# A fused mixing and two-layer kernel: TensorE's program without a loop, and the softmax of the mixing weights in pieces over two blocks

## What is computed

```python
# 1. mixing: softmax over K=7 taps for each token and each of 8 heads, then a causal weighted sum
w = exp(weight_gen - max_k(weight_gen)); w = w / (sum_k(w) + 1e-9)     # [B, S, 8, 7]
x[t, head, :] = sum_k w[t, head, k] * x_pad[t + k, head, :]            # 24 features a head
# 2. layer 1, d_ff = 2048: h = x @ w_in
P = a0 + a1*h + a2*h**2 + a3*h**3;  Q = 1 + |b0|*|h| + |b1|*h**2
x = (P / (Q + 1e-6)) @ w_out
# 3. layer 2, d_ff = 2048: h = x @ w_in2
y = (h * clip(h + 3, 0, 6) / 6) @ w_out2
```

## Time and profile before

| | us |
|---|---|
| median of 3 runs | 1297.59 |
| lowest and highest run | 1291.99, 1297.89 |
| profiled execution, its own time | 1295.64 |
| span of the profiled execution | 1293.9 |
| TensorE busy (matmuls) | 1198.3 |
| VectorE busy | 1204.2 |
| ScalarE busy | 1187.1 |
| GpSimd busy | 1091.9 |
| mean granted TensorE clock | 0.983 |

### The profile page before, as it was taken

The page is one execution under the profiler, slowest core; times in us unless marked ns, Lnnn a source line. Parts: engine busy times, 40 slices in busy tenths (PEclk is TensorE's granted clock), DMA queues, the critical chain, the costliest instruction groups (busy, mean ns, idle before and its releaser), DMA issues.

```text
span 1293.9 us, 19407 instructions
## 1 busy us (share of the span) xinstructions
PE 1198.3 (93%) x5128; PEld 967.6 (75%) x5128; DVE 1204.2 (93%) x1898; ACT 1187.1 (92%) x2221; POOL 1091.9 (84%) x817
## 2 busy tenths in 40 slices
PE   2456899999999999999899999999999999999998
PEld 1344678887888778887688878887788888888876
DVE  5689999999999999999899999999999999999932
ACT  3878999999999999999799999999999999999954
POOL 5878979897998979898797979989798989965554
PEclk9679999999999999999999999999999999999999
DMA  5443222321322322140223213123221302000000
GB/s 168 99 118 78 69 61 50 81 54 38 75 48 61 74 61 49 50 83 28 61 50 85 49 40 75 46 61 74 61 50 52 76 26 54 13 17 1 13 13 13
DMA packets 61464, 73.62 MB, mean 57 GB/s; under 512 B 15912, under 2 KB 42280, under 8 KB 61096
## 3 DMA queue, kind: packets, MB, share of 16 engines
q1 hardware_dynamic: 61352, 72.35, 24.2%
HBM read 56.44 MB, written 8.01 MB: 50 GB/s over the span
## 4 chain that ended last, share of the span: by engine, by line
PE 60%; DVE 22%; issue 11%; ACT 6%; DMA 1%; SPq 0%; POOLq 0%; POOL 0%; ACTq 0%; DVEq 0%
PE h L653 6%; PE h L657 6%; PE h L656 6%; PE h L654 6%; PE h L655 6%; PE acc L661 6%; PE acc L662 6%; PE acc L665 6%; PE acc L664 6%; PE acc L663 6%; DVE early L1031 5%; DVE early L1025 4%; DVE early L1056 4%; DVE early L1019 3%; DVE q_recip L1040 3%
## 5 line engine op out<-in xcount | busy, mean ns | idle before, releaser
L592 POOL TENSOR_TENSOR g_lo<-early,g_hi 128x512 fp32r<-128x512 f32 x256 | 333.3, 1302 | 116.2 <-ACT g_hi L847 107.2
L601 POOL TENSOR_TENSOR g_lo<-late,g_hi 128x512 fp32r<-128x512 f32 x256 | 333.4, 1303 | 23.7 <-ACT g_hi L867 23.7
L653 PE MATMUL h<-x_hi,w_in_hi 128*128 128x512 f32 x512 | 209.1, 408 | 64.1 <-DVE early L1056 61.7
L1064 DVE SCALAR_TENSOR_TENSOR late<-late,h 128x512 f32<-128x512 f32 x256 | 174.5, 682 | 42.8 <-ACT late L858 40.0
L661 PE MATMUL acc<-g_hi,w_out 128*128 128x512 f32 x512 | 202.6, 396 | 5.1 <-DVE late L1076 3.0
L654 PE MATMUL h<-x_lo,w_in_hi 128*128 128x512 f32 x512 | 202.1, 395 | 0.0
L657 PE MATMUL h<-x_tail_lo,w_in_tail 128*128 128x512 f32 x512 | 202.0, 394 | 0.0
L656 PE MATMUL h<-x_tail_hi,w_in_tail 128*128 128x512 f32 x512 | 201.7, 394 | 0.0
L655 PE MATMUL h<-x_hi,w_in_lo 128*128 128x512 f32 x512 | 201.7, 394 | 0.0
L662 PE MATMUL acc<-g_hi,w_out 128*128 128x512 f32 x512 | 201.2, 393 | 0.0
L663 PE MATMUL acc<-g_lo,w_out 128*128 128x512 f32 x512 | 200.7, 392 | 0.0
(11 more groups left out here) (87 smaller groups left out, 2464.2 us busy)
## 6 DMA issues: line engine op xcount, KB each, us to landing
mix_w<-mix_weights SPq DMA_DIRECT2D x75, 192.0 KB
mix_w<-mix_weights SPq DMA_DIRECT2D x75, 144.0 KB
x_win<-in_x SPq DMA_DIRECT2D x15, 393.0 KB, 3.4
mix_w<-mix_weights SPq DMA_DIRECT2D x60, 96.0 KB
mix_w<-mix_weights SPq DMA_DIRECT2D x60, 72.0 KB
out_y<-late SPq DMA_DIRECT2D x16, 256.0 KB, 2.0
x_tail_hi<-tail_hi SPq DMA_DIRECT2D x60, 64.0 KB, 2.0
x_tail_lo<-tail_lo SPq DMA_DIRECT2D x60, 64.0 KB, 2.0
```

Source lines behind the costliest of these rows:

```text
L592: nc.gpsimd.tensor_tensor(g1_lo[p][:, :], neg_g[p], g1_hi[p][:, :].bitcast(F32), ALU.subtract).then_inc(g1_lo_ready, 1)
L601: nc.gpsimd.tensor_tensor(g2_lo[p][:, :], gate[p], g2_hi[p][:, :].bitcast(F32), ALU.subtract).then_inc(g2_lo_ready, 1)
L653: pe.matmul(out[:, :], w_hi[:, cols], hi[:, :], start=True, stop=False)
```

## The change

TensorE's program is written out for all 18 segments, as the others are: `segments`, `Fori` and the register in the counts go.

The softmax of a part p from 3 on is spread over two segments. In the odd one before: maximum of a fourth of the part (16 tokens, 128x112 to 128x16) on VectorE at each of c=4, 6, 8 and 10, subtraction at c=13. In the even one: exp at c=0; the sum over taps on GpSimd, six additions of 128x64 at c=4 to 9 and the 1e-9 at c=10, each waiting for the one before it; the reciprocal on VectorE in two halves of 128x32 at c=12 and 13; the scaling at c=15. Part 2 is done in segment 0, with the scaling at c=1 of segment 1. SyncE loads a part behind the store of the one before it, no longer at the start of its own segment.

```diff
-        def segments(eng, segment):
-            for s in range(FIRST, LOOP_FROM):
-                segment(0, s)
-            with eng.Fori(0, LOOPS) as turn:
-                for s in range(LOOP_FROM, LOOP_FROM + LOOP_BLOCKS):
-                    segment(turn, s)
-            for s in range(LOOP_FROM + LOOP_BLOCKS * LOOPS, LAST + 1):
-                segment(0, s)
...
-            segments(pe, segment)
+            all_segments(segment)
...
-        def part_steps(s, at):
-            part = (s + 4) // 2
-            return {at: part} if s >= 0 and s % 2 == 0 and part < PARTS else {}
-
-        MAX_AT, SUB_AT, EXP_AT, SUM_AT, SCALE_AT = 7, 10, 10, 11, 14
+        EARLY_STEPS = {"max": {4: (0,), 6: (1,), 8: (2,), 10: (3,)}, "sub": {13: (0,)}}
+        LATE_STEPS = {"exp": {0: (0,)}, "sum": {4: (1,), 5: (2,), 6: (3,), 7: (4,), 8: (5,), 9: (6,), 10: (7,)},
+                      "recip": {12: (0,), 13: (1,)}, "scale": {15: (0,)}}
+        THIRD_EARLY = {"max": {6: (0, 1), 7: (2, 3)}, "sub": {10: (0,)}, "exp": {10: (0,)},
+                       "sum": {12: (1, 2, 3), 13: (4, 5, 6, 7)}, "recip": {14: (0,), 15: (1,)}}
+        THIRD_LATE = {"scale": {1: (0,)}}
+
+        def part_steps(s, step, c):
+            found = []
+            if s == 0:
+                found = [(2, THIRD_EARLY)]
+            elif s == 1:
+                found = [(2, THIRD_LATE), (3, EARLY_STEPS)]
+            elif s > 1:
+                found = [(s // 2 + 3, EARLY_STEPS) if s % 2 else (s // 2 + 2, LATE_STEPS)]
+            return [(part, k) for part, steps in found if part < PARTS for k in steps.get(step, {}).get(c, ())]
...
-                for part in part_steps(s, 0).values():
-                    if part == 2:
-
-                        sp.wait_ge(out_lo[1], 8)
-                    load_gen(part)
+                if s == 0:
+
+                    sp.wait_ge(out_lo[1], 8)
+                    load_gen(2)
...
-                for part in part_steps(s, 0).values():
+                part = s // 2 + 2
+                if s >= 0 and s % 2 == 0 and part < PARTS:
                     sp.wait_ge(gen_scaled, part + 1)
                     store_gen(part)
                     sp.wait_ge(gen_stored[part], 16 * H)
+                    if part + 1 < PARTS:
+                        load_gen(part + 1)
...
+            def sum_tap(part, k):
+                if k == 1:
+                    pool.wait_ge(gen_exp, part + 1)
+                else:
+                    pool.wait_ge(gen_sum, sum_count(part, k - 1))
+                stat = gen_stat(part)
+                if k == K:
+                    nc.gpsimd.tensor_scalar(stat, stat, 1e-9, None, ALU.add).then_inc(gen_sum, 1)
+                else:
+                    so_far = gen_w(part)[:, 0, :] if k == 1 else stat
+                    nc.gpsimd.tensor_tensor(stat, so_far, gen_w(part)[:, k, :], ALU.add).then_inc(gen_sum, 1)
...
+            def max_fourth(part, i):
+                if i == 0:
+                    dve.wait_ge(gen_loaded[part], 16)
+                cols = fourth(part_tokens(part), i)
+                dve.tensor_reduce(gen_stat(part)[:, cols], over_k(gen_w(part))[:, cols, :], AX_X,
+                                  ALU.max).then_inc(gen_max, 1)
+
+            def recip_half(part, half):
+                if half == 0:
+                    dve.wait_ge(gen_sum, sum_count(part))
+                n = part_tokens(part) // 2
+                stat = gen_stat(part)[:, half * n:(half + 1) * n]
+                dve.reciprocal(stat, stat).then_inc(gen_recip, 1)
```

More of the change, by code:

```diff
@@ L249, in build_program, with count @@
         x2_tail_lo_ready = sem("x2_tail_lo_ready")
-        def count(turn, per, block, more):
-            return turn * (LOOP_BLOCKS * per) + (block * per + more)
+        def count(per, block, more):
+            return block * per + more
         def all_segments(segment):
             for s in range(FIRST, LAST + 1):
-                segment(0, s)
-        def segments(eng, segment):
-            for s in range(FIRST, LOOP_FROM):
-                segment(0, s)
-            with eng.Fori(0, LOOPS) as turn:
-                for s in range(LOOP_FROM, LOOP_FROM + LOOP_BLOCKS):
-                    segment(turn, s)
-            for s in range(LOOP_FROM + LOOP_BLOCKS * LOOPS, LAST + 1):
-                segment(0, s)
+                segment(s)
         def has1(s, c, back=0):
@@ L409, in _ @@
             sp.wait_ge(gen_stored[0], 16 * H)
-            load_mix_w(0, 1, slice(0, A_TAPS), mix_w_a)
+            load_mix_w(1, slice(0, A_TAPS), mix_w_a)
             sp.wait_ge(in1_tail_lo, 4)
@@ L417, in _, with mix_done, copy_tail @@
             sp.wait_ge(gen_stored[1], 16 * H)
[L418 to L424, removed]
+            load_mix_w(1, slice(A_TAPS, K), mix_w_b)
+            def mix_done(blk, taps):
+                sp.wait_ge(mix_product_ready, count(K, blk - 1, taps))
+            def copy_tail(blk):
                 hi, lo = x1[blk % 2][2], x1[blk % 2][3]
-                sp.wait_ge(x1_tail_hi_ready, count(turn, 1, blk, 0))
+                sp.wait_ge(x1_tail_hi_ready, count(1, blk, 0))
                 for rows in (0, D2):
@@ L435, in copy_tail, with segment @@
                                      tail_lo[half * D2:(half + 1) * D2, :].bitcast(F32)).then_inc(tail_lo_copied, 16)
-            def segment(turn, s):
+            def segment(s):
                 if s == -1:
@@ L630, in prepare @@
                         split_out(1, i, (slot1, slot0)[i // 2])
[L631 to L632 removed]
+                    for part, _ in part_steps(s, "sub", c):
+                        subtract_max(part)
+                    for part, k in part_steps(s, "sum", c):
+                        sum_tap(part, k)
                     if n == 2:
                         scale(1)
[L635 to L636 removed]
+                    for part, _ in part_steps(s, "scale", c):
+                        scale(part)
                 for c in range(NC):
@@ L916, in prepare @@
                         exp_gen(1)
-                    if c in part_steps(s, EXP_AT):
-                        exp_gen(part_steps(s, EXP_AT)[c])
+                    for part, _ in part_steps(s, "exp", c):
+                        exp_gen(part)
                 for c in range(NC):
```

229 lines of the change are left out of this document (115 added, 114 removed).

## The result

The changed kernel takes 1279.26 us (median of 4 runs, 1277.9 to 1279.63) against 1294.79 (4 runs, 1291.76 to 1297.89). The ratio is 0.9885, with a 95% interval of 0.9867 to 0.9903. The forecast was 1277.5, with a range of 1271 to 1287. The profiled execution takes 1279.6 us against 1295.64, so 16.0 less where 18.4 were summed up. In a later comparison on another chip the same kernel gives 1277.97 us and a ratio of 0.9871 (0.9849 to 0.9893).

A forecast was written before the change was run, and what follows sets the result against it. TensorE, VectorE and GpSimd were taken as near full, handing work over each step. Five pairs 11.0, segment 0 1.7 and loop 5.7 make 18.4 us; 1295.64 - 18.4 = 1277.2, stated as 1277.5, range 1271 to 1287.

The forecast's parts named there:

- The loop, 5.7 us: TensorE's one backward jump, between segments 6 and 7: removing it gives back 5.7 us.
- The 0 taken as left: Straight-line code where the jump was: 0 of the 5.7 us remains, bounds 0 and 5.7.
- The pieces on VectorE, 1.5 us: Softmax work on VectorE per part: 3.27 us removed, four maxima and two half reciprocals added at 1.5 us.
- The pair, 146.7 us: Two segments, maximum to maximum: 148.9 us falls to 146.7, a gain of 2.2 us, bounds 2.5 and 0.9.
- the prediction's own three steps: Rule that each VectorE piece comes off its lead over TensorE three steps after the piece's own step.
- the walk: VectorE's lead over TensorE followed step by step: 146.4 us a pair with the new pieces, 148.6 with the old placement.
- The sum on GpSimd, 0: Seven added 128x64 operations at 0.3 us, 2.1 us per even segment: GpSimd's lead absorbs them, nobody waits.
- Waits and queues, 0: Waits of exp, additions and scaling, and SyncE's stores and loads: cost 0.
- Segment 0, 1.7 us: Part 2's softmax in segment 0: 1.8 us of TensorE waiting saved, 0.1 added for maxima, gain 1.7.
- rival of small operations with a high price of their own: Each small VectorE or GpSimd operation costs near 0.45 (or 0.59) us, a pair gives 0.9: 1284 us, chance 0.15.
- the rival of a gap that stays: Gap between segments 6 and 7 is no jump and stays, 5.7 us not won: 1283 us, chance 0.06.
- straight code holding up TensorE: Rival: long straight code outruns what fills TensorE's queue, 5.7 us per gap, slower than before: chance 0.03.

The follow-up runs named there:

- e1_straight: Kernel before with only TensorE's loop written out as straight code: 1290.65 us, ratio 0.997.
- e4_max_whole: Changed kernel with the maximum in one piece at c=7 of the odd segment, not four fourths: 1279.61 us, ratio 0.987.
- e7_max_late: Changed kernel with the maximum in one piece at c=12, subtraction at c=15, exp at c=1 of the even segment: 1276.51 us, ratio 0.9847.
- e6_sum_on_vector: Changed kernel with sum over taps, 1e-9 and reciprocal back on VectorE, together at c=11 of the even segment: 1288.5 us, ratio 0.995.
- e11_subtract_later: e10_halves_late with subtraction moved to c=1 of the even segment, exp to c=2, sum to c=5 to 11: 1278.33 us, ratio 0.9858.
- e10_halves_late: e7_max_late with its maximum cut in two halves, at c=12 and c=14 of the odd segment: 1300.66 us, ratio 1.0045.
- e5_add_on_vector: Changed kernel with the addition of 1e-9 on VectorE at c=12, ahead of the reciprocals, not on GpSimd: 1278.83 us.

## Why the prediction was right, step by step

The direction, the mechanism and the size came out. Of 18.4 us the profiled execution shows 16.0; the medians show 15.5, and 17.7 in the later comparison.

- **The loop, 5.7 us.** Right for the profiled execution (5.7 in e1_straight's comparison), and the place and the cause are shown by moving the jump. But it was one draw: over many runs the loop costs 4.1 us. The forecast used a single gap as if it were fixed, while the spread of the three runs shown, 6 us, already had room for the doubt. That did the forecast no harm, since it took the price of the dear jump off an execution that held this jump. The 0 taken as left was right.
- **The pieces on VectorE, 1.5 us.** Four fourths at 0.27 and two halves at 0.27 make 1.6. The line through two sizes of the reduction was good to 0.02 us an operation. The smaller estimate that the prediction drew from the Trainium skill (VectorE: DVE Perf Modes, The TRN2 errata), 0.18 us for a fourth and 0.9 for all six pieces, does not hold here: a fourth lasts 0.35 us, or 0.27 from start to start, and the six take 1.6.
- **The pair, 146.7 us.** Measured 146.8 to 146.9, with the predicted wait at its predicted step: 0.57 to 0.71 us at c=10 of odd segments against about 0.5, and none at c=13 of even ones, or at c=14, which by the prediction's own three steps is the place that the sum at c=11 had hit. The level itself, though, rests in part on a correction: the walk gave 146.4, and 0.3 was added because it lay 0.3 under the trace in both old cases. Five pairs gave 10.3 us, not 11.0. e4_max_whole, e7_max_late and e6_sum_on_vector came out within 0.2 us of the same walk, e11_subtract_later 0.6 beside it and e10_halves_late 5, both for waits that the walk didn't have; e7_max_late had its wait at c=4, where the walk had put it at c=5.
- **The sum on GpSimd, 0.** Right. 0.28 us an addition, and the least lead that I found was about 0.9 us in both kinds of segment, where 0.9 had been named for the odd and 1.3 for the even one. The even one was mis-sized, because at c=9 five additions lie ahead, and I had counted at c=7.
- **Waits and queues, 0.** Right: no computing engine waits for a load or a store more than before (SyncE's queue does stand for its own stores, 3.0 us at most), and GpSimd's new wait for the second half reciprocal, 0.8 us at most, lies in its slack.
- **Segment 0, 1.7 us.** The mis-sized term in the profiled execution: 0.8. The granted clock is lower in the start-up there, 0.72 and 0.83 in the two stretches of 10 us from 130 on where the kernel before had 0.85 and 1.00; the mean clock between 100 and 180 us is 0.91 and not 0.96. In the repeat of the same kernel it is 0.98, and segment 0 takes 72.07 us, 1.6 less than before. The start is a draw as well, and the first 109 us, for which nothing was summed, took 0.7 us more.

So the forecast missed by 2.4 us in the profiled execution: about 1.6 from the start, where the clock varies from run to run, and 0.7 in the pairs. The rival of small operations with a high price of their own falls by e5_add_on_vector and the rows above, the rival of a gap that stays falls by e1_straight, and no run showed straight code holding up TensorE.

## What to carry to other kernels

Where three engines are nearly full, follow the lead of one over the next from step to step. A piece of extra work costs what the lead lacks when it comes due, so its place counts more than its cutting: an uncut maximum at c=12 beat four fourths at c=4 to 10. Then look at every wait that the late engine feeds, not at the one that shows up today, at the other engines that feed the same wait, and at what is queued behind each new wait: a subtraction placed one step after its input in program order stood 5.7 us, since GpSimd was that far ahead of VectorE in its program. A loop's jump on a full TensorE is worth removing, but price it from many runs.

## What the runs showed of the hardware

- Over one backward jump on TensorE two matmuls started 1.5 to 4.2 us apart, in four profiled executions. At 3.5 and 4.2 us the granted clock fell to 0.60 over the next four us, which cost 1.8 us more; at 1.5 and 2.6 us it stayed at 1.0. All told a jump cost 2.1 (with a second stop of 0.94 us), 2.4, 5.0 and 5.7 us, and 4.1 between the medians of 10 and 19 runs.
- An addition of a constant on VectorE to 128x64 lasts 0.18 to 0.20 us beside an idle GpSimd, and 0.84 to 0.88 where it starts 0.5 us into a GpSimd operation of 1.3 us; it ends 0.05 us behind that one.
- A reduction over seven taps with a stride of 64 elements lasts 0.35 us for 128x112 and 0.97 for 128x448, and 0.27 and 0.89 from its start to the next one's, so four pieces cost 0.2 us more than the whole.
